# Reordered additions, gathers and operand splits around the routed layer of an attention and two-MoE kernel

## What is computed

```python
# attention: B, H, S, D = 2, 8, 768, 64
mask = q_assign[:, :, :, None] == k_assign[:, :, None, :]
scores = np.where(mask, scale * q @ k.T, -1e9)
x = softmax(scores) @ v                      # as 1536 tokens of 512 columns

# routed layer: 8 experts, 512 -> 1024 -> 512, gate = the largest probability
for e in range(8):
    m = expert_idx == e
    out[m] = gate_w[m, None] * (np.maximum(x[m] @ w1[e], 0) @ w2[e])

# dense layer: 8 experts, P normalised over rows and columns 8 times
for e in range(8):
    out2 += P[:, e:e + 1] * (np.maximum(out @ v1[e], 0) @ v2[e])
```

## Time and profile before

| what | us |
|---|---|
| median of 3 runs | 1591.67 (1590.71 to 1593.67) |
| the profiled execution, whole | 1594.29 |
| its span from first to last instruction | 1592.5 |
| TensorE busy in the span | 1568.3 (98%) |
| VectorE busy | 1190.0 (75%) |
| ScalarE busy | 770.6 (48%) |
| GpSimd busy | 263.7 (17%) |

### The profile page before, as it was taken

The page is one execution under the profiler, slowest core; times in us unless marked ns, Lnnn a source line. Parts: engine busy times, 40 slices in busy tenths (PEclk is TensorE's granted clock), DMA queues, the critical chain, the costliest instruction groups (busy, mean ns, idle before and its releaser), DMA issues.

```text
span 1592.5 us, 27473 instructions
## 1 busy us (share of the span) xinstructions
PE 1568.3 (98%) x8404; PEld 1390.7 (87%) x8404; DVE 1190.0 (75%) x2026; ACT 770.6 (48%) x1418; POOL 263.7 (17%) x343
## 2 busy tenths in 40 slices
PE   8999999999999999999999999999999999999998
PEld 7999999778888788989999898989899998989897
DVE  7999999999999976876656666666656566666664
ACT  5777779888888852323232323233232333232321
POOL 2111111342333550000100100010001001100102
PEclk9999999999999999999999999999999999999999
DMA  4222323354344310100110010011001100100002
GB/s 101 61 60 69 79 59 90 86 198 148 143 151 151 106 41 27 40 28 27 47 33 27 29 51 27 27 40 40 27 27 45 35 27 28 52 26 27 27 0 79
DMA packets 123701, 94.92 MB, mean 60 GB/s; under 512 B 66345, under 2 KB 101161, under 8 KB 123633
## 3 DMA queue, kind: packets, MB, share of 16 engines
q1 hardware_dynamic: 120848, 86.01, 17.8%
q0 software_dynamic: 2480, 8.13, 1.5%
q10 hardware_dynamic: 304, 0.05, 0.0%
HBM read 87.88 MB, written 6.29 MB: 59 GB/s over the span
## 4 chain that ended last, share of the span: by engine, by line
PE 88%; DVE 7%; issue 3%; ACT 2%; DVEq 0%; DMA 0%; ACTq 0%; POOL 0%
PE moe_bank L1381 11%; PE moe_bank L1383 11%; PE moe_bank L1382 11%; PE moe_bank L1356 10%; PE moe_bank L1359 10%; PE moe_bank L1358 10%; PE attn_ps_out L447 3%; PE attn_ps_probs_t L428 2%; PE moe_bank L1316 2%; PE moe_bank L1318 2%; PE moe_bank L1317 2%; PE moe_bank L1299 2%; PE moe_bank L1301 2%; PE moe_bank L1300 2%; DVE attn_scores L697 1%
## 5 line engine op out<-in xcount | busy, mean ns | idle before, releaser
L2035 DVE SCALAR_TENSOR_TENSOR all_x<-moe_bank,all_x 128x512 f32<-128x512 f32 x336 | 251.4, 749 | 130.8 <-PE moe_bank L1383 130.2
L1356 PE MATMUL moe_bank<-moe_x_t_hi,all_w_hi 128*128 128x384 f32 x896 | 303.0, 338 | 2.0 <-DVE all_w_lo L889 1.4
L1359 PE MATMUL moe_bank<-moe_x_t_hi,all_w_lo 128*128 128x384 f32 x896 | 302.5, 338 | 0.0
L1381 PE MATMUL moe_bank<-moe_w_hi,moe_h_hi 128*128 128x512 f32 x768 | 302.3, 394 | 0.0
L1358 PE MATMUL moe_bank<-moe_x_t_lo,all_w_hi 128*128 128x384 f32 x896 | 301.1, 336 | 0.0
L1382 PE MATMUL moe_bank<-moe_w_lo,moe_h_hi 128*128 128x512 f32 x768 | 300.5, 391 | 0.0
L1383 PE MATMUL moe_bank<-moe_w_hi,moe_h_lo 128*128 128x512 f32 x672 | 264.5, 394 | 0.0
L1356 PEld LDWEIGHTS moe_bank<-moe_x_t_hi,all_w_hi 128*128 128x128 f32 x896 | 168.4, 188 | 13.4 <-issue 2.0
L1358 PEld LDWEIGHTS moe_bank<-moe_x_t_lo,all_w_hi 128*128 128x128 f32 x896 | 168.4, 188 | 10.0
L1359 PEld LDWEIGHTS moe_bank<-moe_x_t_hi,all_w_lo 128*128 128x128 f32 x896 | 168.2, 188 | 0.0
L2196 POOL TENSOR_TENSOR moe_w_sums<-moe_dense_w_raw 128x256 f32<-128x256 f32 x32 | 24.8, 774 | 842.4 <-DVE all_w_lo L889 842.4
(11 more groups left out here) (339 smaller groups left out, 3071.4 us busy)
## 6 DMA issues: line engine op xcount, KB each, us to landing
all_w_raw<-in_moe_w SPq DMA_DIRECT2D x8, 2048.0 KB, 7.5
moe_w_raw<-in_moe_w SPq DMA_DIRECT2D x8, 2048.0 KB, 8.3
moe_dense_w_raw<-in_moe_w SPq DMA_DIRECT2D x64, 256.0 KB, 2.9
moe_dense_w_raw<-in_moe_w SPq DMA_DIRECT2D x32, 512.0 KB, 3.4
attn_q_raw<-in_q SPq DMA_DIRECT2D x32, 192.0 KB, 3.0
attn_k_raw<-in_k SPq DMA_DIRECT2D x32, 192.0 KB, 3.5
attn_v_raw<-in_v SPq DMA_DIRECT2D x16, 192.0 KB, 3.5
tokens<-all_x SPq DMA_DIRECT2D x32, 96.0 KB, 1.9
```

What stands on the lines that cost most here:

```text
L1356: pe.matmul(out, hi[:, s, k, :], XH[chunk][:, x, k, :], start=(start and k == 0), stop=False, skip_group_check=True)
L1359: mm = pe.matmul(out, lo[:, s, k, :], XH[chunk][:, x, k, :], start=False, stop=(stop and k == 1), skip_group_check=True)
L1381: pe.matmul(out, HH[h][hidden][:, rows], W2H[j][:, f, :], start=(f == 0), stop=False)
L2035: dve.scalar_tensor_tensor(acc, y, PROB[:, row, bass.ds(at, 1)], acc, ALU.mult, ALU.add).then_inc(y_added, 1)
```

## The change

GpSimd's loop is shifted by one turn: `gather(n + 2)` now stands ahead of `add_rows(n - 1)`, where it stood behind it. `add_rows` is cut in two halves of 256 columns. The first half waits until VectorE has split parts 0 and 1 of the next item's second weights (`rw2_lo`), the second half until it has split all four. In the last item VectorE runs `h_part(18, 0)` ahead of `w2_part` 2 and 3, and in `first_tile` a weight split ahead of a reduction. At the seam GpSimd runs `weight_sums(0, 1)` ahead of the last addition and all four sums of pair 5. ScalarE runs `summed_weights(0, 1)` ahead of `hi_parts(3)`, and VectorE runs its own behind the sum `CU3`. TensorE transposes pair 5 ahead of the fourth product of `first_unit`.

```diff
@@ tensor, first_unit
                 multiply(a, 0, 0, S3, T3, False, True).then_inc(chain, 1)
+                transpose_pair(5)
                 pe.wait_ge(copied, 3)
                 multiply(a, 0, 0, A22, T4, False, True).then_inc(chain, 1)
-                transpose_pair(5)
@@ scalar, first_unit
                 act.activation(CP1[:], a, ACT.Copy).then_inc(copied, 1)
+                summed_weights(0, 1)
                 hi_parts(3)
...
                 hi_parts(5)
-                summed_weights(0, 1)
@@ vector, last_tile
+                h_part(n, 0)
                 w2_part(n, r, 2)
                 w2_part(n, r, 3)
-                h_part(n, 0)
@@ vector, first_unit
                 lo_parts(3)
-                token_sums(5)
                 lo_parts(4)
-                low(0, hh, hl, Q11, CP1[:], 1)
                 dve.wait_ge(cross, 1)
                 dve.wait_ge(copied, 3)
                 dve.tensor_tensor(CU3[:], b, CU3[:], ALU.add).then_inc(summed, 1)
+                summed_weights(0, 1)
+                low(0, hh, hl, Q11, CP1[:], 1)
                 low(0, hh, hl, Q22, CU3[:], 2)
                 low(0, hh, hl, Q21, a, 3)
                 lo_parts(5)
-                summed_weights(0, 1)
@@ gpsimd, add_rows
-                pool.tensor_tensor(OUT[:, bass.ds(t, 1), :].rearrange("p o d -> p (o d)"),
-                                   OUTZ[:, bass.ds(s, 1), :].rearrange("p o d -> p (o d)"), Y[n % 2][:], ALU.add
-                                   ).then_inc(ry_added, 1)
+                for half, (cols, done) in enumerate(((slice(0, D // 2), ry_half), (slice(D // 2, D), ry_added))):
+                    if n + 1 < ITEMS:
+                        pool.wait_ge(rw2_lo, W2_PARTS * (n + 1) + 2 * half + 2)
+                    if half == 1:
+                        pool.wait_ge(ry_half, n + 1)
+                    pool.tensor_tensor(OUT[:, bass.ds(t, 1), cols].rearrange("p o d -> p (o d)"),
+                                       OUTZ[:, bass.ds(s, 1), cols].rearrange("p o d -> p (o d)"), Y[n % 2][:, cols],
+                                       ALU.add).then_inc(done, 1)
@@ gpsimd, main loop
-                add_rows(n)
-                if n >= ITEMS - 5 and n < ITEMS - 3:
-                    all_token_sums(n - (ITEMS - 5))
+                else:
+                    add_rows(n - 1)
+                if ITEMS - 4 <= n < ITEMS - 2:
+                    token_sums(n - (ITEMS - 4))
+            add_rows(ITEMS - 3)
             add_rows(ITEMS - 2)
             next_weight_sums()
-            all_token_sums(2)
-            all_token_sums(3)
-            all_token_sums(4)
+            for p in range(2, 5):
+                token_sums(p)
+            weight_sums(0, 1)
             add_rows(ITEMS - 1)
             token_sums(5)
-            weight_sums(0, 1)
```

## The result

The changed kernel takes 1595.58 us (median of 22 runs, 1593.9 to 1597.32), the kernel before 1591.91 us (22 runs beside them, 1590.71 to 1594.95). The ratio is 1.0017, 95% interval 1.0011 to 1.0023: slower by 1.8 to 3.7 us. The forecast was 1593.9 us, +2.2, in a range of 1589.5 to 1597.0. The profiled execution of the changed kernel has a span of 1594.9 us, against 1592.5.

A forecast was written before the change was run, and what follows sets the result against it. The prediction took TensorE to set the pace, with VectorE just keeping up. Its terms, -0.6 + 0 + 0 + 2.4 + 0.4 = +2.2 us, put on the median 1591.67, gave 1593.9 us, range 1589.5 to 1597.0.

The forecast's parts named there:

- Items 2 to 14: Middle of the routed layer: VectorE gains 1.1 us an item, but TensorE waits for nothing there, so 0 us.
- VectorE's pace: Rival: VectorE holds the routed items, so 1.1 us in each of 14 items gives 15.4 us, 1576.3; chance 0.04.
- Item 1: Routed layer's item 1: half additions hinder VectorE's splits less, `h_part(1, 1)` comes earlier; -0.6 us, ends 0 and -0.8.
- Items 15 and 16: Late routed items: waits for hidden rows go, waits at the next weights' split come; 0 us, ends -1.4 and +0.7.
- The last item: End of the routed layer: TensorE's wait before the output and the clock loss go, some 3.7 us, not reaching the end.
- The seam's chain: Into the dense layer: late GpSimd sums hold ScalarE, then VectorE, then pair 4; +2.4 us, ends +0.2 and +4.6.
- shared bandwidth: Alternative to turn-taking at the SBUF port: GpSimd's 2.2 us loss at the seam would be near 0, the sum 0.0.
- Behind pair 4: Pair 4 to the second unit's second product: two waits go, new losses come; about +0.4 us, ends -0.8 and +1.6.
- The 1.0 us for the clock: After pair 4 starts: part of the clock's loss comes back behind a TensorE stand of close to 4 us; 1.0 us.
- Pair 4's pacing: At pair 4 in the seam: VectorE's four low parts set TensorE's pace, 2.2 us for 1.45.
- the unhindered run: Rival at the seam: GpSimd's sums are hardly hindered, pair 4 starts at 573.3; -2.6 us, 1589.1; chance 0.21.
- The longer stand with the clock behind it: Rival: GpSimd gives way for 4.4 us, pair 4 stands longer, half clock adds 1.5; +5.5 us, 1597.2; chance 0.25.

The follow-up runs named there:

- the first experiment: The changed kernel with item 17's addition no longer waiting for the last item's weight splits; 1594.83 us, 1.0007 of the kernel before.
- the second experiment: The changed kernel with ScalarE splitting pair 3's high parts ahead of the second weight sums; 1.0004 of the kernel before.
- the repetition: The kernel before, traced once more with nothing changed; from the routed layer's first product to the first with the second weights 266.02 us, first trace 266.21.

## Right and wrong, step by step

**Items 2 to 14: right.** 1.06 us an item freed on VectorE (1.1 forecast), TensorE's 137.60 us unchanged, so VectorE's pace as a rival is out.

**Item 1: right.** -0.71 us for -0.6.

**Items 15 and 16: right in the mechanism.** The token sums no longer hold the output back, and a wait at the first weights' split came, but once with 0.42 us and not in both items. -0.33 us for 0, inside the ends. So the last item starts 1.04 us earlier for the 0.6 of the forecast.

What follows is counted from the start of the last item (546.87 us before, 546.76 changed), because the forecast's dates from there on are in the time of the kernel before, with the items' gain as a separate term.

**The last item: the step that failed**, by a term that was left out. Low part, wait and clock before the output behaved as said. But the prediction charged only a delay at pair 2, where the stand that makes this delay, 2.36 us, has its own fall of the clock. From the transposes behind the stand to the dense layer's first product it is 5.25 us, and 3.77 in the first experiment, where the clock holds: 1.5 us, in the trace of the second experiment 2.7. Pair 2's sums also ended later, 16.7 us behind the item's start for 15.4 (562.3 - 546.87): with the first weight sums before them they lost 1.1 us beside VectorE, of which this date held nothing. TensorE reached pair 4 3.0 us later than forecast (574.6 us for 571.7) and stood there for 1.47 us, not close to 4. The time of the whole did not suffer from this step, because GpSimd's chain and not TensorE's arrival sets the start of pair 4.

**The seam's chain: right in its links, 0.7 us short in size.** GpSimd starts its sums 9.4 us behind the item's start (9.2 forecast), the second weight sums end at 26.9 (26.1), pair 3's first high part at 28.5 (27.8), and pair 4 starts at 29.3 (28.6): +3.1 us against the kernel before for the +2.4 of the forecast. The mis-sized term is what GpSimd loses to VectorE, 2.9 us for the 2.2 that was put at half of 4.4. What the two engines take fits turn-taking: a sum takes 0.73 us alone and 1.72 us where it stands longest, with values such as 1.19 and 1.60 us between, and a pair of splits takes 2.35 us, or about 0.55 more for each half addition. This agrees with the Trainium skill, "SBUF — State Buffer", section "SBUF: two separate sides", by which one of the two holds the shared port for a whole instruction. That the loss would be near 0 with shared bandwidth, as the prediction has it, no run shows.

**Behind pair 4: mis-sized.** The forecast's own parts (-1.43 - 0.6 + 0.75 + 1.0 + 1.2) come to +0.9 us and not to its +0.4, and its sum would then be +2.7. Measured from pair 4's start to the first product with the second weights it is 11.35 us for 11.93, -0.58. The waits of 1.43 and 0.58 us went and one of 1.35 us came (1.2 forecast). The 1.0 us for the clock did not arise: behind the stand of 1.47 us it stayed at its upper level, as it did behind the stand of 2.42 us in the first experiment. Pair 4's pacing cost 0.41 us (1.85 us from its first transpose to its product, 1.44 before), for 0.75.

**The sum.** -1.04 + 3.10 - 0.58 = +1.48 us in the trace, for -0.6 + 2.4 + 0.4 = +2.2. The errors are -0.4, +0.7 and -1.0 us, so they cancel in part. By the ratio of all times it is +1.8 to +3.7. That the forecast lies between the trace's number and these is partly luck, since nothing in it stands for what the traces lack, which seems to be the kernel before running in some executions without its fall of the clock. Of the rivals, the unhindered run is out (2.9 us were lost), and so is VectorE's pace. The longer stand with the clock behind it came close in time and not in mechanism: the stand and its fall of the clock came at pair 2, before the stand at pair 4, and GpSimd lost 2.9 us and not 4.4.

**What the change does.** Additions in halves are worth 2.0 to 2.2 us by themselves (item 17's free of the last waits), and the low part first adds nothing to them. Item 17's addition behind the last splits costs 2.5 us with the seam of before, and the seam's new order another 1.0 on top: it puts ScalarE behind GpSimd's run of sums, and the last addition behind it too.

## What to carry to other kernels

When an addition is moved out of a faster engine's way, look at the last one: there is no next item to hide it, and what is queued behind it starts as late as it does. A forecast that removes a stall must charge each wait that takes its place with the clock that such a stall can cost, and then ask whether a later wait hides it. And where two parts of a change remove the same stall, each is worth the whole and the second nothing.

## What the chip showed that I had not expected

The clock's fall can't be told from the length of the stand before it. Stands of 1.90 us before the last item's output (1.86 in the repetition) were followed by 3.6 us at about half, 1.43 us in the same place by none, 2.36 us at pair 2 by 3.5 us in three traces and by more than 6 us in a fourth, and 2.42 us at pair 4 in the first experiment by none. By the estimate from the fastest runs the same stand isn't followed by the same fall in each execution either. Behind the stand of 2.42 us:

```profile
575.00:576.00 1.00, 0.84 (x6) 0.64 (x7) 1.00 (x3) 1.00 (x3) 1.00 (x2) 1.00 0.00 0
576.00:577.00 1.00, 0.97 (x9) 0.88 (x9) 0.69 (x2) 1.00 (x4) 1.00 (x2) 1.00 0.00 0
577.00:578.00 1.00, 1.00 (x8) 1.00 (x7) 1.00 (x3) 1.00 (x3) 0.83 (x2) 1.00 0.00 0
```

And the same sums on GpSimd took 17.5 us when they started late and 19.7 us when they started early, with other operations of VectorE beside them.
